# A sort's digit table shared between two engines, and a new order of the steps around it, in a kernel of retention and two mixtures of experts

## The chip, the cores and the metric

The kernel runs on one core of a Trainium2 chip. The metric is the device time of one execution in microseconds; lower is better. Five engines work side by side, each through its own list of instructions in order: TensorE (PE, products), VectorE (DVE), ScalarE (ACT), GpSimd (POOL), and SyncE (SP), which here only issues transfers. They wait for each other by semaphores.

## What is computed

Three stages, each on the output of the one before:

```python
# 1. retention: per head, over 768 steps, batch 4, 8 heads of 64
state = gamma * state + outer(k[t], v[t]);  y[t] = scale * q[t] @ state
# 2. soft mixture of experts, x: 3072 x 512, 8 experts with 4 slots each
d = softmax(x @ phi, over tokens);  c = softmax(x @ phi, over slots)
slot_out[e] = relu((d.T @ x)[e] @ w1[e]) @ w2[e];  x = c @ slot_out
# 3. noisy top-2 of 8 experts on the new x
noisy = x @ w_gate + log1p(exp(x @ w_noise)) * noise
for the two best experts of each token, with weights from a softmax of the two:
    out[token] += weight * relu(x @ w1b[e]) @ w2b[e]
```

## The kernel before

The tokens of stage 2 lie in 24 tiles of 128. Because x of stage 3 is `c @ slot_out`, with 32 slots, the first product of each expert of stage 3 is folded into a 32 x 1024 matrix, called SW: `sw_product(e)` (P0 to P7) multiplies slot_out with w1b[e] on TensorE as soon as SP's load of that matrix lands. ACT finds each one's size in `sw_sums(e)` (Abs with a sum), POOL takes the maximum over partitions for experts 0 to 3 and for 4 to 7 (`sw_all_sum`), and DVE makes power-of-two scales of it (`sw_scales(0)`, `sw_scales(1)`). ACT then writes the high half in f16 (`sw_high`), DVE the low half (`sw_low`), and TensorE spreads both to all partitions (`sw_spread_parts(e)`) in 16 units, two for each expert. The units go through three PSUM banks in turn, so unit n waits until unit n-3 has been copied to SBUF (`sw_keep`, by ACT for units 0 to 7 and the even ones after, by DVE for 9, 11, 13 and 15; `sw_kept` says on which semaphore to wait).

Beside this the routing is worked out. Each of the 6144 (token, choice) pairs gets a position in 55 tiles of 128 rows, ordered by expert. Positions are turned into a gather list, idx, by a counting sort on TensorE: DVE splits each position into a high digit (0 to 54) and a low digit (0 to 127), makes one-hot tables of both (`eq_all` and `eq_hi` of the high, `eq_lo` of the low in three parts of 16 columns of pairs, 128x2048 each), and `sort_rows(0)` to `sort_rows(2)` multiply them, 16 products each, into bank 7. Three small DVE operations make idx of it. The records of all pairs (c in f16, weight, output row) have been written to DRAM by POOL before. When idx and the second all-reduce of SW are there, POOL issues `fetch_records(0)` to `(10)`, one indirect DMA for each tile.

DVE also works out in which order the experts' w2b are used (`order_expert`, with `order_ready`). SP waits for it at the end of its list of loads, to load w2b of the third expert, 2 MB (`load_w2b(EARLY)`, L463); later ones wait for tiles too.

Then the 55 tiles: ACT stages the record's c (`stage_c`, L1102), TensorE turns it (`turn_c`, L898), ACT copies it (`keep_ct`, L1108), `hidden_b` (L921) multiplies with SW, ACT and DVE take the positive part as high and low f16 (`h_high` L1113, `h_low` L1546), `out_b` (L938) multiplies with w2b, 24 products of 512 columns a tile, DVE scales (`keep_y` L1560) and POOL writes (L576) and adds (L582) rows to the output.

Each engine's order is written out by hand. Around the change it is, on TensorE: P6, sort_rows(0), P7, units 0 to 3, sort_rows(1) and (2), units 4 to 7, units 8 and 9, turn_c(0), units 10 to 15, hidden_b(0). On ACT: sw_sums(2) to (5), the scaled eq_hi (L1088), sw_high(0) to (3), sw_sums(6) and (7), copies of units 0 to 7, sw_high(4) to (7), stage_c(0), unit 8, keep_ct(0), stage_c(1), units 10, 12, 14, h_high(0). On DVE: digits (L1479), eq_all, eq_hi, sw_scales(0), eq_lo[0], sw_low(0) to (3), eq_lo[1] and [2] (L1491), idx (L1499 to L1503), sw_scales(1), the order (L1508 to L1514), sw_low(4), and so on. On POOL: records to DRAM, two all-reduces (L560), the fetches (L570).

Of the kernel before, what the change touches and what calls it, by code (L numbers as in the profile page):

```python
# [5 lines left out]
P = 128  # L6
F32 = mybir.dt.float32
F16 = mybir.dt.float16
I32 = mybir.dt.int32
ALU = mybir.AluOpType  # L10
# [5 lines left out]
def build_program(nc, chunks, phi, w1a, w2a, w_gate, w_noise, noise, w1b, w2b, consts, out, dims):  # L16
# [3 lines left out]
    NT = B * NC  # L20
# [36 lines left out]
    with ExitStack() as ctx:  # L57
        def sb(name, shape, dt):
            return ctx.enter_context(nc.sbuf_tensor(name, shape, dt))

        def sem(name):
            return ctx.enter_context(nc.semaphore(name))
# [147 lines left out]
        digit = sb("digit", [P, 2, 2 * NT], F16)  # L210
        count_i = r_region[:, 4 * SZ + 2 * E * NT:4 * SZ + 2 * E * NT + P].bitcast(I32)
# [115 lines left out]
        eq_lo_ready = sem("eq_lo_ready")  # L327
        idx_done = sem("idx_done")
# [55 lines left out]
        def sw_kept(unit):  # L384

            if unit < 8 or unit % 2 == 0:
                return sw_act_kept, unit + 1 if unit < 8 else unit // 2 + 5
            return sw_dve_kept, (unit - 7) // 2
# [117 lines left out]
        def _(pool):  # L506
# [55 lines left out]

            for group in SW_GROUPS:
                sw_all_sum(*group)
# [22 lines left out]
            top = pool.to_reg(TOP)  # L587
# [23 lines left out]
        def _(pe):  # L611
# [251 lines left out]
            def sort_rows(part):  # L863
                if part == 0:
                    pe.wait_ge(eq_hi_ready, 1)
                    pe.wait_ge(eq_row_ready, 1)
                pe.wait_ge(eq_lo_ready, part + 1)
                for j in range(part * LO_PART, (part + 1) * LO_PART):
                    last = nc.tensor.matmul(bank[7][:, 0:2 * RT], eq_lo[part][:, j % LO_PART, :], eq_hi[:, j, :, :].rearrange("p v i -> p (v i)"),
                                            start=(j == 0), stop=(j == 2 * NT - 1), skip_group_check=True)  # L870
                if part == 2 * NT // LO_PART - 1:
                    last.then_inc(idx_done, 1)
# [14 lines left out]
            sw_product(7)  # L887
# [4 lines left out]
            sort_rows(2)  # L892
            sw_spread_parts(2)
# [87 lines left out]
        def _(act):  # L981
# [102 lines left out]
            for e in range(2, 6):  # L1084
                sw_sums(e)

# [5 lines left out]
            sw_sums(6)  # L1092
            sw_sums(7)
            for unit in range(8):
                sw_keep(unit)
            act.wait_ge(sw_scale_ready, 2)
            for e in range(4, E):
                sw_high(e)

# [20 lines left out]
            stage_c(1, 1, rec_arrival(1))  # L1120
            for unit in range(10, 2 * E, 2):
                sw_keep(unit)
            h_high(0, 0)
# [26 lines left out]
        def _(dve):  # L1150
# [328 lines left out]
            link(nc.vector.tensor_copy(digit[:, :, :], digit_i[:, :, :, :].rearrange("p d k t -> p d (k t)")))  # L1479
            by_hi = [P, 2 * NT, RT]  # L1480
# [9 lines left out]
            for j in range(0, 2 * NT, LO_PART):  # L1490
# [3 lines left out]
                if j == 0:  # L1494
                    for e in range(4):
                        sw_low(e)

            dve.wait_ge(idx_done, 1)
# [8 lines left out]
            numbers = count[0:1, 0:E]  # L1507
            link(nc.vector.tensor_reduce(order_e[:, 0, :], ahead[0:1, :, :], AX_X, ALU.add))  # L1508
            pairs = ahead_tiles[0:1, :, :]
            link(nc.vector.tensor_tensor(pairs, order_e[:, 0, :].unsqueeze(1).to_broadcast([1, E, E]),  # L1510
                                         numbers.unsqueeze(2).to_broadcast([1, E, E]), ALU.is_equal))
            link(nc.vector.tensor_tensor(pairs, pairs, numbers.unsqueeze(1).to_broadcast([1, E, E]), ALU.mult))
            link(nc.vector.tensor_reduce(order_e[:, 1, :], pairs, AX_X, ALU.add))
            nc.vector.tensor_copy(order_expert[:, :], order_e[:, 1, :]).then_inc(order_ready, 1)  # L1514
            dve.wait_ge(order_ready, 1)
# [142 lines left out]
```

## Time and profile before

| | us |
|---|---|
| median of 3 runs | 578.58 |
| lowest and highest | 577.02, 579.87 |
| the profiled execution | 580.67 |
| its span, first to last instruction | 578.9 |
| TensorE busy | 516.4 (89%) |
| VectorE busy | 284.0 (49%) |
| ScalarE busy | 188.8 (33%) |
| GpSimd busy | 254.6 (44%) |

Times in the rows are microseconds from the span's start. A row of the timeline gives start, duration, engine, line and operation, what is written and read, how many instructions were merged (x16), and in brackets how long the engine had been idle and what released it. DMA-issuing instructions of SP have the engine name SPq. In the chain of waits each row is a start, a duration and what the end of the kernel waited for in that time.

### The profile page before, as it was taken

To read this page: it belongs to the slowest core of one execution; us is meant where nothing else is said; L and a number is where in the kernel's file an instruction comes from. 1 tells how busy PE (TensorE), PEld (TensorE's weight loads), DVE (VectorE), ACT (ScalarE), POOL (GpSimd) and SP (SyncE) were. 2 spreads that over 40 slices of the span, in tenths; PEclk is the share of its full clock that TensorE was granted. 3 is DMA by queue.
4 is the path that set the end of the run, shared out by engine and by line. 5 is a ranking of instruction groups with operands and counts; after the bars stand their busy time and mean duration, and the time that the engine had idled before them with its cause. 6 is when DMAs were issued, how large, how long until landed. Compare 5 with 4: busy or idle time off the path is not lost.

```text
span 578.9 us, 13504 instructions
## 1 busy us (share of the span) xinstructions
PE 516.4 (89%) x4845; PEld 305.9 (53%) x4846; DVE 284.0 (49%) x450; ACT 188.8 (33%) x353; POOL 254.6 (44%) x216
## 2 busy tenths in 40 slices
PE   4999999997876746469999999999999999999993
PEld 4787787774474524324545454554545454545441
DVE  1666666565570488357345464546452423233330
ACT  0222222221830123546363645455322221212120
POOL 1222211211000010525558687868676666656542
PEclk9999999999985797759999999999999999999997
DMA  8899899877999996442445522222132333333410
GB/s 277 312 367 371 304 378 327 331 290 288 407 426 427 426 428 279 155 148 60 181 171 199 188 51 45 42 40 55 26 56 47 50 46 51 45 50 43 53 18 1
DMA packets 29621, 107.90 MB, mean 186 GB/s; under 512 B 11251, under 2 KB 12515, under 8 KB 24464
## 3 DMA queue, kind: packets, MB, share of 16 engines
q1 hardware_dynamic: 15408, 92.89, 41.7%
q0 software_dynamic: 14176, 14.49, 14.3%
q8 instruction: 26, 0.43, 0.3%
q14 instruction: 11, 0.09, 0.1%
HBM read 93.87 MB, written 29.43 MB: 213 GB/s over the span
## 4 chain that ended last, share of the span: by engine, by line
PE 77%; DMA 12%; DVE 4%; issue 2%; ACT 1%; another core or an unknown queue 1%; POOL 1%; SPq 0%; DVEq 0%; POOLq 0%
PE ps L938 49%; DMA w_region<-moe_w 9%; PE ps L670 4%; PE ps L921 4%; PE ps L623 4%; PE ps L664 4%; PE ps L655 3%; PE ps L677 2%; DMA s_region<-moe_w 1%; PE ps L644 1%; PE ps L808 1%; PE ps L637 1%; DMA rec_region<-records,idx 1%; PE ps L844 1%
## 5 line engine op out<-in xcount | busy, mean ns | idle before, releaser
L938 PE MATMUL ps<-w_region,s_region 128*128 (+1 forms) x1320 | 297.1, 382 | 3.7 <-ACT s_region L1113 3.6
L938 PEld LDWEIGHTS ps<-w_region,s_region 128*128 128x128 f16 x1320 | 127.2, 98 | 149.5 <-issue 10.0
L1546 DVE SCALAR_TENSOR_TENSOR s_region<-ps,s_region 128x1024 f16<-128x1024 f32 x55 | 67.4, 1225 | 156.3 <-ACT s_region L1113 150.9
L1113 ACT ACTIVATE s_region<-ps 128x1024 f16<-128x1024 f32 x55 | 56.3, 1023 | 194.7 <-PE ps L921 136.8
L576 POOL DMA_INDIRECT out<-s_region,rec_region x41 | 54.5, 1330 | 53.5 <-DVE s_region L1560 51.5
L582 POOL DMA_INDIRECT out<-s_region,rec_region x42 | 67.8, 1615 | 15.2 <-issue 12.3
L570 POOL DMA_INDIRECT rec_region<-records,idx x55 | 57.6, 1047 | 20.4 <-issue 20.4
L511 POOL TENSOR_TENSOR s_region<-w_region,s_region 128x512 f32<-128x512 f32 x22 | 22.9, 1042 | 89.2 <-PE ps L677 73.7
L921 PEld LDWEIGHTS ps<-s_region,sw_region 128*128 (+1 forms) x440 | 29.5, 98 | 14.9 <-issue 2.1
L1560 DVE TENSOR_SCALAR s_region<-ps,rec_region,y_scale 128x512 f32<-128x512 f32 x42 | 33.8, 804 | 5.7 <-PE ps L938 4.1
L921 PE MATMUL ps<-s_region,sw_region 128*128 128x128 f16 x440 | 34.0, 221 | 1.7 <-issue 1.7
L1161 DVE TENSOR_TENSOR sw_region<-ps,s_region 128x512 f32<-128x512 f32 x24 | 16.6, 691 | 34.2 <-PE ps L670 34.2
L1332 DVE SCALAR_TENSOR_TENSOR w_region<-w_region,w2b_scale 128x2048 f16<-128x2048 f32 x12 | 28.0, 2345 | 2.1 <-ACT w_region L1024 2.1
L808 PE MATMUL ps<-w_region,sw_region 128*32 128x128 f32 x448 | 19.2, 348 | 8.1 <-DMA w_region<-moe_w 7.6
L844 PE MATMUL ps<-w_region,slot_out_t 128*32 128x256 f32 x224 | 17.5, 465 | 10.1 <-DMA w_region<-moe_w 9.5
L576 POOL DMA_INDIRECT out<-r_region,rec_region x13 | 18.2, 1401 | 17.6 <-DVE r_region L1560 16.8
L1024 ACT ACTIVATE w_region<-w_region,w2b_scale 128x2048 f16<-128x2048 f32 x12 | 23.8, 2001 | 4.3 <-DVE w2b_scale L1326 4.3
L556 POOL DMA_DIRECT2D records<-rec_region x1 | 0.7, 742 | 53.4 <-DVE rec_region L1457 53.4
L984 ACT ACTIVATE s_region<-ps 128x128 f32<-128x128 f32 x24 | 6.7, 277 | 51.9 <-PE ps L637 51.9
L1039 ACT ACTIVATE r_region<-w_region 128x2048 f16<-128x2048 f32 (+1 forms) x14 | 23.3, 1666 | 0.1
L582 POOL DMA_INDIRECT out<-r_region,rec_region x13 | 20.7, 1592 | 4.5 <-issue 4.5
L808 PEld LDWEIGHTS ps<-w_region,sw_region 128*32 128x32 f32 x448 | 16.8, 141 | 10.5 <-DMA w_region<-moe_w 9.2
(239 smaller groups left out, 589.6 us busy)
## 6 DMA issues: line engine op xcount, KB each, us to landing
w_region<-moe_w SPq DMA_DIRECT2D x19, 2048.0 KB, 23.4
w_region<-chunks SPq DMA_DIRECT2D x34, 512.0 KB, 6.6
w_region<-moe_w SPq DMA_DIRECT2D x14, 1024.0 KB, 8.8
sw_region<-chunks SPq DMA_DIRECT2D x12, 512.0 KB, 6.2
s_region<-moe_w SPq DMA_DIRECT2D x3, 2048.0 KB, 22.0
s_region<-moe_w SPq DMA_DIRECT2D x2, 1024.0 KB, 8.2
s_region<-moe_w SPq DMA_DIRECT2D x1, 1536.0 KB, 6.4
out<-s_region,rec_region POOLq DMA_INDIRECT x83
```

What stands on the lines that cost most here:

```text
L570: nc.gpsimd.indirect_dma_start(rec_i[:, i * RW:(i + 1) * RW], None, records[:, :], bass.IndirectOffsetOnAxis(ap=idx[:, i:i + 1], axis=0), ...
L576: nc.gpsimd.indirect_dma_start(out[:, :], bass.IndirectOffsetOnAxis(ap=rec_i[:, i * RW + SL + 1:i * RW + SL + 2], axis=0), y_sb[i % DEPTH] ...
L582: nc.gpsimd.indirect_dma_start(out[:, :], bass.IndirectOffsetOnAxis(ap=rec_i[:, i * RW + SL + 2:i * RW + SL + 3], axis=0), y_sb[i % DEPTH] ...
L808: last = nc.tensor.matmul(bank[5][j * SL:(j + 1) * SL, 0:P], h1_blocks[:, at:at + SL], w[:, f, j * P:(j + 1) * P], start=(e == 0 and f == ...
L921: last = nc.tensor.matmul(bank[2 + 2 * r + f // 4][:, f % 4 * P:(f % 4 + 1) * P], sw_parts[:, bass.ds(e, 1), f * P:(f + 1) * P].rearrange( ...
L938: last = nc.tensor.matmul(bank[6 + r], h[:, r, f, :], w2b_parts[:, bass.ds(o, 1), part, f, :].rearrange("p e m -> p (e m)"), start=(first ...
L1024: nc.scalar.activation(w2b_parts[:, e, 0, chunks, :], w2b_in[e].rearrange("p (c m) -> p c m", c=FC)[:, chunks, :], ACT.Copy, scale=w2b_sca ...
L1039: nc.scalar.activation(unused, w2b_in[e][:, part * UNIT // parts:(part + 1) * UNIT // parts], ACT.Abs, accum_out=w2b_sum[:, 0, e, part:par ...
L1113: nc.scalar.activation(h_hi[:, r, :, :].rearrange("p c t -> p (c t)").rearrange("p (a n) -> p a n", a=2), ps[:, 2 + 2 * r:4 + 2 * r, :], A ...
L1332: last = nc.vector.scalar_tensor_tensor(out=w2b_parts[:, e, 1, chunks, :], in0=w2b_in[e].rearrange("p (c m) -> p c m", c=FC)[:, chunks, :] ...
L1546: nc.vector.scalar_tensor_tensor(out=h_lo[:, r, :, :].rearrange("p c t -> p (c t)").rearrange("p (a n) -> p a n", a=2), in0=ps[:, 2 + 2 * ...
L1560: nc.vector.tensor_scalar(y_sb[r], bank[6 + u % 2], rec[:, bass.ds(i * RW + SL, 1)], y_scale[:, bass.ds(o, 1)], ALU.mult, ALU.mult).then_i ...
```

## The change

- DVE makes parts 0 and 1 of the low digit's table. Part 2 is made on ACT: for each of its 16 columns |count - digit| in f16 (Abs with the negated digit as bias), then Relu(1 - that) over all 2048, which is 1 where the two are equal. DVE writes the negated digits (`digit_minus`); three new semaphores join the two. On ACT this stands between sw_sums(4) and sw_sums(5).
- TensorE: sw_product(7) moves from ahead of units 0 to 3 to behind sort_rows(2).
- ACT: the copies of units 0 to 3 stand ahead of sw_sums(7), unit 4 behind it, unit 6 behind sw_high(7). Units 5 and 7 are copied by DVE, behind sw_scales(1).
- DVE: the five operations of the experts' order stand ahead of the wait for the sort.
- ACT: stage_c(1) stands behind the copies of units 10, 12 and 14.
- POOL: the register load of TOP stands ahead of the wait for idx.

```diff
-            if unit < 8 or unit % 2 == 0:
-                return sw_act_kept, unit + 1 if unit < 8 else unit // 2 + 5
-            return sw_dve_kept, (unit - 7) // 2
+            if unit < 4 or unit % 2 == 0:
+                return sw_act_kept, unit + 1 if unit < 4 else unit // 2 + 3
+            return sw_dve_kept, (unit - 3) // 2
...
+            top = pool.to_reg(TOP)
             for group in SW_GROUPS:
                 sw_all_sum(*group)
...
-            top = pool.to_reg(TOP)
             for i in range(2 * DEPTH + 3):
                 fetch_records(i)
...
-                pe.wait_ge(eq_lo_ready, part + 1)
+                if part < 2:
+                    pe.wait_ge(eq_lo_ready, part + 1)
+                else:
+                    pe.wait_ge(eq_last_ready, 1)
...
             sort_rows(0)
-            sw_product(7)
             pe.wait_ge(sw_lo_ready, 4)
             sw_spread_parts(0)
             sw_spread_parts(1)
             sort_rows(1)
             sort_rows(2)
+            sw_product(7)
             sw_spread_parts(2)
             sw_spread_parts(3)
...
-            for e in range(2, 6):
+            for e in range(2, 5):
                 sw_sums(e)
+
+            act.wait_ge(digits_ready, 1)
+            for j in range(LO_PART):
+                last = nc.scalar.activation(eq_lo[2][:, j, :], count[:, :], ACT.Abs, bias=digit_minus[:, j:j + 1])
+            last.then_inc(gaps_ready, 1)
+            act.wait_ge(gaps_ready, 1)
+            nc.scalar.activation(eq_lo[2], eq_lo[2], ACT.Relu, scale=-1.0, bias=1.0).then_inc(eq_last_ready, 1)
+            sw_sums(5)
...
             sw_sums(6)
+            for unit in range(4):
+                sw_keep(unit)
             sw_sums(7)
-            for unit in range(8):
-                sw_keep(unit)
+            sw_keep(4)
             act.wait_ge(sw_scale_ready, 2)
             for e in range(4, E):
                 sw_high(e)
+            sw_keep(6)
...
             keep_ct(0, 0)
-            stage_c(1, 1, rec_arrival(1))
             for unit in range(10, 2 * E, 2):
                 sw_keep(unit)
+            stage_c(1, 1, rec_arrival(1))
...
+            nc.vector.tensor_scalar(digit_minus[:, :], digit[:, 0, 2 * LO_PART:3 * LO_PART], -1.0, None,
+                                    ALU.mult).then_inc(digits_ready, 1)
...
-            for j in range(0, 2 * NT, LO_PART):
+            for j in range(0, 2 * LO_PART, LO_PART):
...
-            dve.wait_ge(idx_done, 1)
...
-            sw_scales(1)
             numbers = count[0:1, 0:E]
...
             dve.wait_ge(order_ready, 1)
+            dve.wait_ge(idx_done, 1)
...
+            sw_scales(1)
+            sw_keep(5)
+            sw_keep(7)
             sw_low(4)
```

## Rows read from the trace of the kernel before

**Rows 1.** The page, the chain that ended last, by engine and by line
```profile
PE 77%; DMA 12%; DVE 4%; issue 2%; ACT 1%; another core or an unknown queue 1%; POOL 1%; SPq 0%; DVEq 0%; POOLq 0%
PE ps L938 49%; DMA w_region<-moe_w 9%; PE ps L670 4%; PE ps L921 4%; PE ps L623 4%; PE ps L664 4%; PE ps L655 3%; PE ps L677 2%; DMA s_region<-moe_w 1%; PE ps L644 1%; PE ps L808 1%; PE ps L637 1%; DMA rec_region<-records,idx 1%; PE ps L844 1%
```
**Rows 2.** The chain of waits in order of time: start, us, what
```profile
237.55 6.83 DMA rec_region<-records,idx
...
246.95 5.06 another core or an unknown queue
252.04 1.03 ACT s_region L1113
253.21 6.26 PE ps L938 x16
259.97 5.18 PE ps L938 x24
```
**Rows 3.** The timeline of TensorE, 223 to 249
```profile
223.30 2.57 PE L844 MATMUL ps<-w_region,slot_out_t 128*32 128x256 f32 x32 [2.26 <-DMA w_region<-moe_w]
225.80 1.65 PE L869 MATMUL ps<-r_region,s_region 128*128 128x110 f16 x16
229.19 1.93 PE L844 MATMUL ps<-w_region,slot_out_t 128*32 128x256 f32 x32 [1.74 <-DMA w_region<-moe_w]
231.05 0.85 PE L857 MATMUL ps<-s_region,r_region 128*64 128x256 f16 x12
...
232.53 1.78 PE L869 MATMUL ps<-r_region,sw_region 128*128 128x110 f16 x32
...
239.95 1.49 PE L857 MATMUL ps<-s_region,r_region 128*64 128x256 f16 x12
245.25 1.49 PE L857 MATMUL ps<-s_region,r_region 128*64 128x256 f16 x12 [3.81 <-ACT sw_region L1061]
248.45 1.01 PE L921 MATMUL ps<-s_region,sw_region 128*128 128x128 f16 x8 [1.71 <-issue]
```
**Rows 4.** The timeline of VectorE, 215 to 248
```profile
215.03 0.21 DVE L1479 CAST digit<-r_region 128x96 f16<-128x96 int32 x1
...
226.33 4.48 DVE L1491 TENSOR_TENSOR sw_region<-count,digit 128x2048 f16<-128x2048 f16 x2
...
234.85 0.21 DVE L1503 SCALAR_TENSOR_TENSOR idx<-ps,r_region 128x55 int32<-128x55 f32 x1
...
236.62 0.16 DVE L1514 CAST order_expert<-order_e 1x8 int32<-1x8 f32 x1
...
241.66 0.47 DVE L1466 SCALAR_TENSOR_TENSOR s_region<-ps,sw_scale,s_region 128x256 f16<-128x256 f32 x1
...
247.66 0.69 DVE L1473 CAST sw_region<-ps 128x512 f16<-128x512 f32 x1 [1.04 <-issue]
```
**Rows 5.** The timeline of ScalarE, 221 to 240
```profile
221.09 0.38 ACT L1051 ACTIVATE s_region<-ps 128x256 f32<-128x256 f32 x1 [6.11 <-PE ps L844]
...
221.46 2.54 ACT L1088 ACTIVATE r_region<-s_region,row 128x2640 f16<-128x2640 f16 x1
223.90 1.55 ACT L1055 ACTIVATE s_region<-ps,sw_scale 128x256 f16<-128x256 f32 x4
...
239.30 0.31 ACT L1102 ACTIVATE s_region<-rec_region 128x128 f16<-128x128 f16 x1 [1.09 <-DMA rec_region<-records,idx]
```
**Rows 6.** The timeline of GpSimd and of SyncE's queue, 231 to 238
```profile
231.74 0.38 POOL L560 PARTITION_ALL_REDUCE sw_sum<-sw_sum  x1 [13.41 <-ACT s_region L1051]
236.10 1.14 POOL L570 DMA_INDIRECT rec_region<-records,idx  x1 [3.98 <-issue]
...
237.81 0.35 SPq L463 DMA_DIRECT2D w_region<-moe_w  x1
```
**Rows 7.** Stretches: us; busy PE, PEld, DVE, ACT, POOL; PEclk; DMA share; GB/s
```profile
228.00:236.00 8.00, 6.02 (x96) 4.18 (x96) 4.25 (x11) 3.73 (x9) 0.38 (x1) 1.00 0.01 2
...
242.00:244.00 2.00, 0.00 (x0) 0.00 (x0) 0.14 (x1) 0.00 (x0) 1.45 (x2) 0.50 1.01 428
```
**Rows 8.** Groups of ScalarE's instructions by line: busy, mean ns, idle before
```profile
L1078 ACT ACT_TABLE_LOAD x1 | 1.3, 1283 | 0.0
```

More of the change, by code:

```diff
@@ L210, in build_program @@
         digit = sb("digit", [P, 2, 2 * NT], F16)
+        digit_minus = sb("digit_minus", [P, LO_PART], F32)
         count_i = r_region[:, 4 * SZ + 2 * E * NT:4 * SZ + 2 * E * NT + P].bitcast(I32)
@@ L327, in build_program @@
         eq_lo_ready = sem("eq_lo_ready")
+        digits_ready = sem("digits_ready")
+        gaps_ready = sem("gaps_ready")
+        eq_last_ready = sem("eq_last_ready")
         idx_done = sem("idx_done")
@@ L1496, in _ @@
                         sw_low(e)
-            dve.wait_ge(idx_done, 1)
-            link(nc.vector.tensor_scalar(idx_part[:, 0, :], bank[7][:, 0:RT], 0.0, float(RECORDS + 2 * NT), ALU.is_equal,
-                                         ALU.mult))
-            link(nc.vector.scalar_tensor_tensor(out=idx_part[:, 1, :], in0=bank[7][:, 0:RT], scalar=float(2 * NT),
-                                                in1=idx_part[:, 0, :], op0=ALU.mult, op1=ALU.add))
-            nc.vector.scalar_tensor_tensor(out=idx[:, :], in0=bank[7][:, RT:2 * RT], scalar=-float(2 * NT),
-                                           in1=idx_part[:, 1, :], op0=ALU.add, op1=ALU.add).then_inc(idx_ready, 1)
-            sw_scales(1)
             numbers = count[0:1, 0:E]
@@ L1515, in _ @@
             dve.wait_ge(order_ready, 1)
+            dve.wait_ge(idx_done, 1)
+            link(nc.vector.tensor_scalar(idx_part[:, 0, :], bank[7][:, 0:RT], 0.0, float(RECORDS + 2 * NT), ALU.is_equal,
+                                         ALU.mult))
+            link(nc.vector.scalar_tensor_tensor(out=idx_part[:, 1, :], in0=bank[7][:, 0:RT], scalar=float(2 * NT),
+                                                in1=idx_part[:, 0, :], op0=ALU.mult, op1=ALU.add))
+            nc.vector.scalar_tensor_tensor(out=idx[:, :], in0=bank[7][:, RT:2 * RT], scalar=-float(2 * NT),
+                                           in1=idx_part[:, 1, :], op0=ALU.add, op1=ALU.add).then_inc(idx_ready, 1)
+            sw_scales(1)
+            sw_keep(5)
+            sw_keep(7)
             sw_low(4)
```

## Prediction

> **What bounds the kernel now.** I read the page first: of the chain that ended last, 77% is TensorE and 49% L938 alone, the product of the output tiles [rows 1]. Its 55 tiles run back to back from the first one on (24 products in 5.18 us from 259.97, and so on to the end [rows 2]), so whatever moves the start of tile 0's L938 moves the end by as much, and nothing else in this change touches what follows. Next I read the chain of waits in order of time, ahead of that start: record 1's fetch (6.83 us), then 5.06 us that end in no release that the profile can name, then ACT's L1113 (h_high of tile 0), then L938 at 253.21 [rows 2]. Then the four engines and SP from 214 to 253, instruction by instruction. The reader is to see a queue that is held at its head: ACT issues in order, and its stage_c(1) stands ahead of the copies of units 10, 12 and 14. Record 1 lands at 237.55 + 6.83 = 244.38, though unit 10 was through TensorE when the group of 239.95 had done its first four products. TensorE restarts the last three units only at 245.25 and reaches hidden_b(0) (L921) at 248.45 [rows 3]. Ahead of that, the sort ends at 232.53 + 1.78 = 234.31 [rows 3], DVE makes idx by 235.06 [rows 4], POOL starts fetch 0 at 236.10 and record 0 is used at 239.30 [rows 5, 6].
>
> **The last third of the digit table on ACT.** DVE loses one of the two L1491 of the pair at 226.33, 2.24 us [rows 4], and gains one 128x16 negation of about 0.1 to 0.2 us right after the digit copy of 215.03 [rows 4]. ACT gains 16 Abs of 128 columns, a wait on itself, and one Relu of 2048 columns. It has idled 6.11 us up to 221.09 [rows 5], for w1b[5]'s product. Start: digits at 215.03 + 0.21, the negation, so 215.5. No row has this Abs with its bias. The nearest are stage_c, 0.31 us for 128 columns alone, and the four L1055 with a scale operand, 1.55 us for four of 256 columns, 0.39 each. Back-to-back ones overlap, so the bounds are 0.19 (half of the wider one) and 0.39; I take 0.28, a little under the row of the same width: 16 x 0.28 = 4.5, to 220.0. Relu: 2.54 x 2048/2640 = 1.97 by L1088 [rows 5], to 222.0. So sw_sums(5) starts 0.9 us late; by the bounds the table ends at 220.5 (no delay) to 223.7 (2.6 late). The Trainium skill, ScalarE: Activation LUTs, What ACT_TABLE_LOAD costs, says that a pointer operand for the bias adds about 93 ns and that neighbours overlap by as much; by its figures an estimate for one Abs is 0.29 us, and the sum would not change.
>
> Who waits behind it: L1088, the four sw_high of 223.90, DVE's sw_low, and DVE's second table, whose end moves from 228.57 to 229.5. Part 3's table (222.0) is no longer late for anyone.
>
> **Sort ahead of P7.** Here P6 and P7 are sw_product(6) and (7). TensorE finished sort_rows(0) at 227.45 and stood idle until w1b[7] landed, 1.74 us before 229.19 [rows 3]. In the new order it does units 0 to 3 there. Units 0 to 2 take 0.85 and unit 3 another 0.41 after a copy by ACT, as at 231.05 [rows 3], now at 227.45 to about 229.2, part of it at the lower clock. The second table ends at 229.5, so sorts 1 and 2 run 229.5 to 231.3 (1.78, at full clock: 1.00 from 228 to 236 [rows 7]). DVE's three index operations end 235.06 - 234.31 = 0.75 after the sort: idx at 232.0, against 235.06, 3.1 us earlier. The cost: P7 moves from 229.19 to 231.3 and ends at 233.2 (1.93). POOL's second all-reduce stands ahead of the fetches in its queue and needs sw_sums(7). In before it began 0.62 us after P7's end and took 0.38 [rows 3, 6]. Now that gives 234.2. So 2.2 of the 3.1 us are lost to POOL's queue. From there POOL needs 236.10 - 235.06 = 1.04 to its first fetch [rows 4, 6]; moving the register load of TOP ahead can take at most a part of that, and I count nothing: fetch 0 starts at 235.2, 0.9 earlier.
>
> **Order of experts in DVE's wait.** From idx's end at 235.06 to 236.78 DVE does nine small operations, the four of sw_scales(1) and the five of this order, so the five take some 1.0 us, now beside TensorE's sort: order_ready at 229.5 + 1.0 = 230.5 instead of 236.78 [rows 4]. Nothing on DVE waits for them. But SP has been waiting for this semaphore, and 1.03 us later, at 237.81, issued the 2 MB load of the third expert's w2b [rows 6]. It will now go at 231.5. In before the DMA engines were still full of it at 242 to 244, at 428 GB/s [rows 7], and record 1, asked for at 237.55, fell under it: 6.83 us from issue to landing, where record 0 took 239.30 - 236.10 = 3.2 including the start of stage_c. By that the load's data will now lie at about 232 to 238, so **record 0 falls under its tail**. Two readings of its landing: free of the load, 235.2 + 3.2 = 238.4; as record 1, which came 244.38 - 237.81 = 6.57 after the load's issue, 231.5 + 6.6 = 238.1. The upper bound is the whole 6.8: 242.0. I take 238.8, a little over the two that agree, so stage_c(0) gains 0.5 us (bounds: +1.4 with a table that costs no delay, to -2.7).
>
> **Copies shared anew, and stage_c(1) behind SW's copies.** Units 5 and 7 go to DVE at 0.69 each and ACT takes unit 6 behind the second sw_high. ACT's last sw_high ends about 236.7 by this plan (scales ready by 235.0, 1.59 for the four as in the group of rows 5), so units 8 and 9 are through before record 0 arrives. From stage_c(0) on, the order is that of before: units 10 to 12 start 0.65 after it (239.95 against 239.30). Then keep(10) follows at once, where before it waited for record 1. In the old clock: unit 10 done about 240.6, its copy to 241.2, unit 13 to 241.9; sw_low(7), 241.66 + 0.47 = 242.13 [rows 4], then lets unit 14 run to 242.6 and, with unit 12's copy, unit 15 to 243.05. In before they ended at 245.25 + 1.49 = 246.74 [rows 3]. That takes 3.7 us off. Record 1, fetched 1.45 us after record 0, is not needed until ACT has copied unit 14, some 4 us later, and even a 6.8 us fetch would reach h_high by less than a microsecond.
>
> **The unnamed waits.** Unit 15's products end at 246.74 but DVE's copy of it starts at 247.66, with "issue" as the only reason [rows 4]: 0.92 us. hidden_b(0) ends at 248.45 + 1.01 = 249.46, but L1113 starts at 252.04 [rows 2, 3]: 2.58 us. The change gives no reason why they should go, and the traces none why they should stay. The profiled execution took 580.67 against a median of 578.58, 2.1 more, so the timed runs may not have them in either kernel. Both ways they cancel. Bounds: 0 and 3.5 us of further gain.
>
> **The sum.** 0.5 (record 0) + 3.7 (record 1's hold gone) = 4.2 us, tile 0's L938 at 249.0 instead of 253.2. The first L938 group took 6.26 us for 16 products 0.39 each (the clock stood at 0.50, the 1.2 GHz level, at 242 to 244 [rows 7]), where the rest take 0.22. TensorE works in the same pattern ahead of it, so I count this as equal, within 1 us either way. The profiled 580.67 becomes 576.5 with a span of 574.7; applied to the median, 578.58 - 4.2 = **574.4 us**.
>
> **Rivals.**
> 1. Record 0 is held by the early w2b load as record 1 was, 6.8 us: at 242.0, stage_c(0) loses 2.7 where I count a gain of 0.5, and it stands ahead of everything else on ACT. 574.4 + 3.2 = 577.6: no change that can be told. For it: record 1 shows the effect at full size. Against it: the load will be 3.7 us old at the fetch, not 0.3 us younger.
> 2. The unnamed waits go with the new timing, in runs that had them: 3.5 us more, 570.9. For it: nothing else ended so late there. Against: no cause is known.
> 3. A small transfer is served in turn with the large one: record 0 is free of the load, at 238.4 or, with no delay by ACT's table, 237.9: 573.5 to 574. The Trainium skill, DMA: Bandwidth & Descriptors, Queues, rings and completion order, states that each DMA engine goes round its queues packet by packet, which would make an overlap cheap. The 6.83 us against 3.2 in the trace speak against it, so this gets little.
> 4. Slower: ACT's table overruns. Place: between 215.5 and P5's sums. If Abs, Relu and the return to Abs each cost a table load of 1.28 us [rows 8], and one Abs 0.39, the table ends at 215.5 + 3.8 + 6.2 + 2.0 = 227.5, 6.4 us late instead of 0.9. Sort, order, P7 and fetches shift by the 5.5 us more, and 4.2 becomes -1.3: 579.9. It decides from a delay of 5.1 us on, slower from there. By over 0.5% it would need a delay of 8 us. Against it: Abs, Copy and Relu ran before with no load between them.
>
> **Chances.** Forecast 0.45 (572.9 to 576), rival 1 0.22, rival 2 0.18, rival 3 0.10, rival 4 0.05. A measurement here tells a change from about 0.5%, 2.9 us: below 575.7 is faster. Of the forecast's cases some 0.85 lie there, of rival 1's 0.2, all of rivals 2 and 3: 0.38 + 0.04 + 0.18 + 0.10 = 0.70 faster. Slower by over 0.5% only with an overrun beyond rival 4's or a fault of a kind that I don't see: 0.04; the same: 0.26. The range leaves out half of rival 4 and the outer parts of rivals 1 and 2: 570.5 to 577.8.
>
> **What would show it.** ACT's Abs group ends by about 220 and Relu by 222, or else step one is off. Sort's end at 231.3 and idx at 232.0; P7 at 231.3; first L570 at 235.2, released by the all-reduce. L463 at 231.5, with the DMA rate high from 232 on. Landing of record 0 (start of L1102) decides between the forecast, rivals 1 and 3. No ACT idle of microseconds between stage_c(0) and unit 14. L1113 at 247.9, or 244.4 if rival 2 holds. The prediction is wrong if record 0 waits out the load's whole length, or if a new wait stands ahead of fetch 0.

## Result: 3.1 us faster, and the profile after

| | before | changed |
|---|---|---|
| median of 8 runs, us | 578.36 | 575.26 |
| lowest and highest | 576.83, 580.91 | 572.91, 576.31 |
| the profiled execution | 580.67 | 572.91 |
| its span | 578.9 | 571.2 |

The ratio of the times is 0.9935, 95% interval 0.9909 to 0.9960. The medians are 3.1 us apart (2.3 to 5.3 by the interval), where 4.2 had been forecast. The profiled executions are 7.8 us apart, more than twice as much. That of before is near the slow end of its kernel's runs and that of the changed kernel is the fastest of its own, so the profiles are read here by distances inside one execution. In the changed kernel's profile the work ahead of the change (the digit copy of DVE, 215.83 against 215.03) came 0.8 us later; distances from that copy leave this out. They hold for these two executions only: in the kernel before the path to the fetch doesn't start at that copy, but at the landing of w1b[7], for which P7 waits [rows 3]. The sections on run 9 and on the sum come back to this.

The timeline of ScalarE in the changed kernel (start, us, engine, line; L1096 is the Abs, L1099 the Relu, L1058 sw_sums, L1103 the scaled eq_hi, L1062 sw_high, L1068 the copies, L1119 stage_c, L1125 keep_ct, L1130 h_high):

```profile
216.28 4.78 ACT L1096 ACTIVATE sw_region<-count,digit_minus 128x128 f16<-128x128 f16 x16 [0.77 <-DVE digit_minus L1497]
221.10 1.91 ACT L1099 ACTIVATE sw_region<-sw_region 128x2048 f16<-128x2048 f16 x1
222.91 0.36 ACT L1058 ACTIVATE s_region<-ps 128x256 f32<-128x256 f32 x1
...
240.73 0.31 ACT L1119 ACTIVATE s_region<-rec_region 128x128 f16<-128x128 f16 x1 [2.69 <-DMA rec_region<-records,idx]
240.94 0.58 ACT L1068 ACTIVATE sw_region<-ps 128x512 f16<-128x512 f32 x1
241.48 0.28 ACT L1125 ACTIVATE s_region<-ps 128x128 f16<-128x128 f16 x1
242.06 0.60 ACT L1068 ACTIVATE sw_region<-ps 128x512 f16<-128x512 f32 x1 [0.30 <-PE ps L861]
...
246.11 1.02 ACT L1130 ACTIVATE s_region<-ps 128x1024 f16<-128x1024 f32 x1 [1.01 <-PE ps L928]
```

Against [rows 5]: the 6.11 us of idle time ahead of sw_sums(5) are filled with the table. Record 0 is used (stage_c(0)) at 240.73, against 239.30, and now ACT waits 2.69 us for it. Then nothing holds the queue: the copy of unit 10 comes 0.3 us after keep_ct, and h_high(0) starts 5.38 us after stage_c(0), where before it took 12.74.

TensorE of the changed kernel, in its new order (L848 P6 and P7, L876 the sort, L861 units, L928 hidden_b, L945 out_b):

```profile
224.12 3.51 PE L848 MATMUL ps<-w_region,slot_out_t 128*32 128x256 f32 x32 [2.44 <-DMA w_region<-moe_w]
227.56 0.98 PE L876 MATMUL ps<-r_region,s_region 128*128 128x110 f16 x16
228.47 0.84 PE L861 MATMUL ps<-s_region,r_region 128*64 128x256 f16 x12
...
230.47 1.78 PE L876 MATMUL ps<-r_region,sw_region 128*128 128x110 f16 x32 [0.49 <-DVE sw_region L1510]
232.19 1.93 PE L848 MATMUL ps<-w_region,slot_out_t 128*32 128x256 f32 x32
...
245.46 0.61 PE L928 MATMUL ps<-s_region,sw_region 128*128 128x128 f16 x8 [0.84 <-ACT sw_region L1068]
...
247.28 5.30 PE L945 MATMUL ps<-w_region,s_region 128*128 128x512 f16 x16 [1.15 <-ACT s_region L1130]
```

Against [rows 3], the idle 1.74 us ahead of P7 are used, the sort waits 0.49 us for DVE's second table, and P7 comes last. DVE's end of idx, POOL and SP's queue:

```profile
232.87 0.21 DVE L1531 SCALAR_TENSOR_TENSOR idx<-ps,r_region 128x55 int32<-128x55 f32 x1
```
```profile
234.75 0.38 POOL L564 PARTITION_ALL_REDUCE sw_sum<-sw_sum  x1 [15.54 <-ACT s_region L1058]
235.64 1.15 POOL L575 DMA_INDIRECT rec_region<-records,idx  x1 [0.51 <-issue]
```
```profile
232.49 15.79 SPq L467 DMA_DIRECT2D w_region<-moe_w  x2
```

Idx is ready at 233.08, but POOL first does the all-reduce that needs P7, so the fetch starts 2.6 us after idx (1.04 before, [rows 4, 6]). The load (L467, two issues merged in this row) now goes 3.15 us ahead of the first fetch. The chain of waits names what follows:

```profile
235.64 5.06 DMA rec_region<-records,idx
240.70 0.02 issue
240.73 0.32 ACT s_region L1119
```

Record 0 takes 5.06 us from fetch to landing and 5.09 to its use, where it took 3.2 to its use before. The stretches (busy PE, PEld, DVE, ACT, POOL; PEclk; DMA share; GB/s) show what the DMA engines did meanwhile:

```profile
234.00:236.00 2.00, 1.30 (x20) 0.72 (x16) 0.73 (x5) 0.97 (x4) 0.74 (x2) 1.00 0.67 262
236.00:238.00 2.00, 0.43 (x4) 0.18 (x4) 1.91 (x4) 2.00 (x5) 1.69 (x2) 0.90 0.96 410
238.00:240.00 2.00, 0.73 (x6) 0.19 (x4) 1.08 (x2) 0.04 (x1) 1.39 (x3) 0.50 0.68 282
```
The last of these stretches, cut in two, and the next:

```profile
238.00:239.00 1.00, 0.73 (x6) 0.19 (x4) 0.23 (x1) 0.04 (x1) 0.70 (x2) 0.50 1.15 492
239.00:240.00 1.00, 0.00 (x0) 0.00 (x0) 0.86 (x2) 0.00 (x0) 0.69 (x2) 0.50 0.21 72
240.00:242.00 2.00, 0.82 (x7) 0.64 (x9) 0.00 (x0) 1.03 (x3) 1.70 (x2) 0.50 0.20 20
```

The load's traffic is over at 239.0, 6.5 us after its issue. Record 0 lands at 240.70, 1.7 us behind that.

### The profile page after: what moved, and what is told of

It is laid out like the page before. It is cut to its first block, busy times and chain, and to the rows that moved or that the text cites. A ratio compares the mean times of both kernels' runs of the same rounds, so it can differ in the third digit from the quotient of the medians.

```text
span 571.2 us, 13520 instructions
## 1 busy us (share of the span) xinstructions
PE 514.7 (90%) x4845; PEld 302.8 (53%) x4846; DVE 282.9 (50%) x452; ACT 194.7 (34%) x368; POOL 255.0 (45%) x216
## 4 chain that ended last, share of the span: by engine, by line
PE 75%; issue 14%; DMA 3%; DVE 2%; ACT 2%; POOL 2%; SPq 0%; DVEq 0%; POOLq 0%
PE ps L945 49%; PE ps L674 4%; PE ps L928 4%; PE ps L627 4%; PE ps L668 4%; PE ps L659 3%; PE ps L681 2%; ACT r_region L1046 1%; DMA s_region<-moe_w 1%; PE ps L648 1%; PE ps L641 1%; DMA rec_region<-records,idx 1%; PE ps L703 1%; DMA w_region<-chunks 1%; DVE s_region L1190 1%
## 5 line engine op out<-in xcount | busy, mean ns | idle before, releaser
L945 PE MATMUL ps<-w_region,s_region 128*128 (+1 forms) x1320 | 295.6, 381 | 1.1 <-ACT s_region L1130 1.1
L945 PEld LDWEIGHTS ps<-w_region,s_region 128*128 128x128 f16 x1320 | 127.2, 98 | 145.3 <-issue 3.6
L1130 ACT ACTIVATE s_region<-ps 128x1024 f16<-128x1024 f32 x55 | 56.3, 1023 | 188.9 <-PE ps L928 184.6
L928 PEld LDWEIGHTS ps<-s_region,sw_region 128*128 (+1 forms) x440 | 29.1, 98 | 13.9 <-ACT sw_region L1068 1.2
L928 PE MATMUL ps<-s_region,sw_region 128*128 128x128 f16 x440 | 33.5, 219 | 0.8 <-ACT sw_region L1068 0.8
L1178 DVE TENSOR_TENSOR sw_region<-ps,s_region 128x512 f32<-128x512 f32 x24 | 16.6, 691 | 34.2 <-PE ps L674 34.2
L848 PE MATMUL ps<-w_region,slot_out_t 128*32 128x256 f32 x224 | 19.7, 513 | 6.9 <-DMA w_region<-moe_w 6.4
L812 PE MATMUL ps<-w_region,sw_region 128*32 128x128 f32 x448 | 15.8, 302 | 9.7 <-DMA w_region<-moe_w 9.1
L1171 DVE TENSOR_TENSOR sw_region<-ps,s_region 128x512 f32<-128x512 f32 x24 | 15.4, 680 | 9.6 <-PE ps L627 9.6
```

The lines of the kernel that those rows point to most:

```text
L928: last = nc.tensor.matmul(bank[2 + 2 * r + f // 4][:, f % 4 * P:(f % 4 + 1) * P], sw_parts[:, bass.ds(e, 1), f * P:(f + 1) * P].rearrange( ...
L945: last = nc.tensor.matmul(bank[6 + r], h[:, r, f, :], w2b_parts[:, bass.ds(o, 1), part, f, :].rearrange("p e m -> p (e m)"), start=(first ...
L1130: nc.scalar.activation(h_hi[:, r, :, :].rearrange("p c t -> p (c t)").rearrange("p (a n) -> p a n", a=2), ps[:, 2 + 2 * r:4 + 2 * r, :], A ...
```

## The experiments

The theory after the result: the gain is the removal of record 1's hold on ACT's queue, which SP's w2b load had caused. That hold could be removed in two ways, and the change does both: it moves stage_c(1), and it issues the load early enough for records 0 and 1 to land together. The earlier sort and fetch are given back, because the same early load now delays record 0. The rivals: the earlier sort and fetch are the gain; or the two profiles differ mostly by the unnamed waits.

Times are medians. A ratio and its interval are taken from all the runs of both kernels, so a ratio is not quite the quotient of two medians.

| run | us | its before | ratio, 95% interval |
|---|---|---|---|
| 1, before, stage_c(1) moved | 574.86 | 578.28 | 0.9938 (0.9910 to 0.9966) |
| 2, changed, stage_c(1) back | 574.29 | 578.28 | 0.9937 (0.9911 to 0.9964) |
| 3, changed, load behind record 0 | 573.14 | 578.28 | 0.9926 (0.9894 to 0.9957) |
| 4, before, order moved | 577.64 | 578.28 | 0.9979 (0.9950 to 1.0008) |
| 5, changed, table on DVE | 575.17 | 578.87 | 0.9928 (0.9897 to 0.9960) |
| 6, before, load behind record 1 | 575.15 | 578.87 | 0.9949 (0.9922 to 0.9975) |
| 7, run 3 and sw_low(7) first | 572.51 | 578.87 | 0.9897 (0.9857 to 0.9938) |
| 8, changed, P7 back | 575.79 | 578.87 | 0.9953 (0.9928 to 0.9979) |
| 10, run 1 and load behind record 0 | 578.47 | 581.21 | 0.9954 (0.9918 to 0.9991) |
| 11, changed again | 579.19 | 581.21 | 0.9983 (0.9951 to 1.0015) |
| 12, run 7 again | 576.58 | 581.21 | 0.9950 (0.9913 to 0.9987) |

The last three, and the look at before of run 9, were made on a second chip, where every kernel took 3 to 4 us more; their times are compared with each other only.

**Run 1: stage_c(1) alone, in the kernel before.**

```diff
-            stage_c(1, 1, rec_arrival(1))
             for unit in range(10, 2 * E, 2):
                 sw_keep(unit)
+            stage_c(1, 1, rec_arrival(1))
```

> Kernel before, with only stage_c(1) moved behind the copies of units 10, 12 and 14. Theory (the head of ACT's queue was held by record 1, which the w2b load kept back): everything up to stage_c(0) stays, record 0 used at 239.3, record 1 still lands about 244.4, but unit 10 is copied at once and the copies of 10 to 14 end by 243.3; h_high(0) starts 3.7 us earlier than in the kernel before with its unnamed waits alike, so 574.7 us. Rival (the gain of the whole change comes from the earlier sort and fetch): nothing here, 578.4. Rival (the unnamed waits of 0.9 and 2.6 us ahead of h_high made most of the difference of the two profiles): the medians differ by less than 1 us while the profile may show more.

Measured 574.86, 3.4 us below before. One moved line does what the whole change does. ScalarE of this run (L1102 stage_c, L1061 copies, L1113 h_high):

```profile
240.95 0.31 ACT L1102 ACTIVATE s_region<-rec_region 128x128 f16<-128x128 f16 x1 [0.97 <-DMA rec_region<-records,idx]
...
242.28 0.60 ACT L1061 ACTIVATE sw_region<-ps 128x512 f16<-128x512 f32 x1 [0.30 <-PE ps L857]
...
246.42 0.31 ACT L1102 ACTIVATE s_region<-rec_region 128x128 f16<-128x128 f16 x1 [1.53 <-DMA rec_region<-records,idx]
246.63 1.00 ACT L1113 ACTIVATE s_region<-ps 128x1024 f16<-128x1024 f32 x1
```

Record 1 is as late as before, 5.5 us behind record 0, but the copies no longer stand behind it. It now holds h_high by 0.7 us: hidden_b(0) had ended at 245.92, and h_high follows record 1 at once.

**Run 2: stage_c(1) put back, in the changed kernel** (run 1's edit reversed).

> Changed kernel, with only stage_c(1) put back ahead of the copies. In the changed kernel records 0 and 1 landed within 0.2 us of each other (240.70 and 240.88), since the w2b load had been issued before both. Theory: stage_c(1) then waits for nothing wherever it stands, and putting it back costs 0.3 us at most: 575.3 to 575.6. Rival (the new place of stage_c(1) carries the gain in the changed kernel too): 3.7 us lost, 579.

Measured 574.29, not above the changed kernel. In its profile both records are there together, so the place of stage_c(1) no longer matters:

```profile
239.54 0.31 ACT L1119 ACTIVATE s_region<-rec_region 128x128 f16<-128x128 f16 x1 [2.73 <-DMA rec_region<-records,idx]
...
240.47 0.30 ACT L1119 ACTIVATE s_region<-rec_region 128x128 f16<-128x128 f16 x1
```

Runs 1 and 2 together: in the kernel before, the place of stage_c(1) is worth the whole gain; in the changed kernel it is worth nothing that can be told.

**Run 3: the load behind record 0, in the changed kernel.**

```diff
                 if o == EARLY:
                     sp.wait_ge(order_ready, 1)
+                    sp.wait_ge(rec_first_full[0], 16)
```

> Changed kernel, with SP's w2b load of the third expert made to wait for record 0's landing as well. Theory (record 0 lands late, 5.1 us after its fetch, because the w2b load issued earlier holds it): record 0 lands 3.2 us after its fetch, about 238.9 instead of 240.7, and the end comes 1.8 us earlier, 573.4. Its price: the load then lands some 6.5 us later, about 247, when ACT wants it at 247.4, so nothing. Rival (record 0's 5.1 us are the fetch's own, with no part of the load): no gain, 575.3; or a loss of up to 1 us if the load is now late.

Measured 573.14, 5.1 us below before. POOL, then ScalarE, of this run:

```profile
234.72 1.14 POOL L576 DMA_INDIRECT rec_region<-records,idx  x1 [0.51 <-issue]
```
```profile
237.78 0.31 ACT L1120 ACTIVATE s_region<-rec_region 128x128 f16<-128x128 f16 x1 [0.66 <-DMA rec_region<-records,idx]
```

Fetch to use is 3.06 us where it was 5.09: the load was the cause of record 0's delay. The time is 2.1 us below the changed kernel's, which the ten runs can't tell for sure; run 7 comes back to it. Not foreseen: the load lands after ACT wants it, and ACT idles 1.81 us ahead of its first sum in this profile; that moves h_high of tile 1, not the copies.

**Run 4: the order of experts alone, in the kernel before.** The five operations from `numbers = ...` to the wait for order_ready stand ahead of `dve.wait_ge(idx_done, 1)`.

> Kernel before, with only the five operations of the experts' order moved ahead of DVE's wait for the sort. Theory: the w2b load is issued about 232.9 instead of 237.8; it now holds record 0 (lands 240.5 to 241 instead of 239.3, 1.4 us lost) but no longer record 1, which lands with it instead of at 244.4. Net 1.5 to 2.5 us faster, 576 to 577, though stage_c(1) still stands ahead of the copies. Rival (the load has no part in record 1's landing): record 1 at 244.4 as before and no change, 578.4. Rival (an earlier load costs record 0 its lead and gives nothing back): 1.4 us slower, 579.8.

Measured 577.64; the interval reaches from 2.9 us faster to 0.5 slower, so the time alone does not choose between the forecast, whose 576 to 577 is just missed, and the first rival. The profile does decide whether the load holds the records: record 0 came 4.83 us after its fetch instead of 3.2, and record 1 was already there 0.93 us later, where before it took 5.1. SP's queue, POOL, ScalarE:

```profile
236.22 0.35 SPq L463 DMA_DIRECT2D w_region<-moe_w  x1
```
```profile
240.57 1.14 POOL L570 DMA_INDIRECT rec_region<-records,idx  x1 [4.05 <-issue]
```
```profile
245.40 0.31 ACT L1102 ACTIVATE s_region<-rec_region 128x128 f16<-128x128 f16 x1 [2.79 <-DMA rec_region<-records,idx]
...
246.33 0.30 ACT L1102 ACTIVATE s_region<-rec_region 128x128 f16<-128x128 f16 x1
```

In this execution P7 took 3.62 us instead of 1.93, because TensorE had the lower clock from 233 to 235 (0.50), so the fetch came some 1.7 us later than it would have.

The early load alone is thus far from the whole gain. Run 2 has the same early load and the same place of stage_c(1), and besides it the rest of the change: the table on ACT, the sort ahead of P7, the new sharing of the copies. It is 3.4 us below run 4. Drawn again and again at random from the recorded runs of both, the difference of the medians lies between 0.7 and 4.9 in 95% of the draws. So the work on the sort and the copies is not worth nothing: it pays for what the early load costs record 0. Which part of it pays, no run shows, for runs 5 and 8 take out one part each and leave the others, and the sharing of the copies was never taken out.

**Run 5: the third part of the table on DVE again, in the changed kernel.** The block of Abs, wait and Relu, the negation and their semaphores go; `range(0, 2 * NT, LO_PART)` returns.

> Changed kernel, with the third part of the digit table made on DVE again (no Abs, Relu or negation; ACT goes straight to sw_sums(5)). Theory: the table on ACT delayed sw_sums(5) by 1.2 us and DVE's second table by as much, so its removal gives that back, and DVE's third table ends about 231.4, 1 us after the second one ends now. The sort ends within 0.3 us of where it does now, order_ready and the w2b load 1 us later, fetch 0 as now: 575.3, within 0.5 either way. Rival (the table on ACT is what makes the sort early, worth the 2.2 us that one table costs DVE): 577.5.

Measured 575.17 against 575.26 for the changed kernel: the table on ACT is worth nothing that can be told. The price that the forecast put on it (ACT late, DVE's second table late) eats what DVE saves: the first fetch comes 19.80 us after the digit copy, and in the changed kernel 19.81. Record 0 is used 1.1 us later after that copy (25.96 against 24.90), since the load now goes only 2.35 us ahead of the fetch; the times don't show it. In the profile the sort's last part waits 0.30 us for DVE's third table:

```profile
231.81 0.98 PE L873 MATMUL ps<-r_region,sw_region 128*128 128x110 f16 x16
233.09 0.98 PE L873 MATMUL ps<-r_region,sw_region 128*128 128x110 f16 x16 [0.30 <-DVE sw_region L1499]
```

**Run 6: the load behind record 1, in the kernel before.** Run 3's line with `rec_first_full[1]`; nothing of the change is in it.

> Kernel before, with nothing changed but that SP's w2b load of the third expert also waits for record 1's landing; stage_c(1) stays ahead of the copies. Theory (that load is what kept record 1 back from 240.8 to 244.4): record 1 lands 3.2 us after its fetch, ACT's queue is held 0.5 us at most, and the end comes 3.2 to 3.7 us earlier: 574.6 to 575.1. Rival (record 1's landing has nothing to do with the load, it comes from fetches that follow one another): 578.3, or later where the load is now late.

Measured 575.15, 3.7 us below before. Another way to the same gain, and the cleanest proof that the load held record 1, which now comes 2.50 us after its fetch. Stage_c of both records, and ACT's first sum over the expert's w2b (L1040), for which it waits:

```profile
241.11 0.31 ACT L1103 ACTIVATE s_region<-rec_region 128x128 f16<-128x128 f16 x1 [0.96 <-DMA rec_region<-records,idx]
...
241.99 0.30 ACT L1103 ACTIVATE s_region<-rec_region 128x128 f16<-128x128 f16 x1
...
251.15 1.91 ACT L1040 ACTIVATE r_region<-w_region 128x2048 f16<-128x2048 f32 x1 [3.26 <-DMA w_region<-moe_w]
```

The late load has a price, which was named with the rival: h_high of tile 1 starts 8.59 us after that of tile 0, where it is 7.33 in run 9's profile of the kernel before. So some 1.3 us of what record 1's release gives are lost again.

**Run 7: run 3 with sw_low(7) ahead of DVE's copy of unit 11.**

```diff
             sw_low(6)
-            sw_keep(11)
             sw_low(7)
+            sw_keep(11)
```

> Changed kernel with the w2b load behind record 0's landing, as in the run that gave 573.1, and with DVE's sw_low(7) ahead of its copy of unit 11. Theory: units 14 and 15 were released by sw_low(7), 0.28 us after unit 13; now by the copies of 11 and 12, 0 to 0.3 us earlier: 572.9, not to be told from 573.1, and clearly below the kernel before. Rival (DVE's order there costs the 0.6 us that a copy takes): 572.5.

Measured 572.51, 6.4 us below before, at the rival's number; 0.6 us from run 3 can't be told apart. The six units 10 to 15 now ran as one group on TensorE (238.49, 2.95 us). It is 2.8 us below the changed kernel (0.4 to 4.9, drawn as above). The gate has its price here too, for ACT waits for the load:

```profile
247.07 1.91 ACT L1047 ACTIVATE r_region<-w_region 128x2048 f16<-128x2048 f32 x1 [2.77 <-DMA w_region<-moe_w]
```

H_high of tile 1 starts 8.10 us after that of tile 0, in the changed kernel 6.95.

**Run 8: P7 ahead of units 0 to 3 again, in the changed kernel.**

```diff
             sort_rows(0)
+            sw_product(7)
             pe.wait_ge(sw_lo_ready, 4)
...
             sort_rows(2)
-            sw_product(7)
```

> Changed kernel, with P7 put back between sort_rows(0) and units 0 to 3. Theory (the first fetch waits in POOL's queue behind the all-reduce that needs P7, so sort and P7 only trade places): the sort ends about 1.8 us later, idx comes about 234.9 instead of 233.1, and is now what releases fetch 0, about 236 instead of 235.6; record 0 lands at most 0.5 us later, since the load's tail ends at the same time: 575.3 to 576. Rival (the sort ahead of P7 is worth the 1.9 us of P7): 577.2.

Measured 575.79, 0.5 us above the changed kernel and not to be told from it. What releases the fetch has changed from the all-reduce to idx, as expected:

```profile
239.93 1.14 POOL L575 DMA_INDIRECT rec_region<-records,idx  x1 [1.68 <-DVE idx L1531]
```

The fetch comes 20.94 us after the digit copy instead of 19.81, 1.1 later, since P7 took 3.24 us here, at the lower clock, instead of 1.93. Record 0 makes good a part of that: its use is 0.8 us later (25.68 against 24.90).

**Run 9: the kernel before, a second profile.**

> The kernel before, unchanged, for a second look at its profile. If the 0.9 us ahead of unit 15's copy and the 2.6 us between hidden_b(0) and h_high(0) belong to the kernel, they stand here too. If they belong to that one execution (none of the eight other profiles so far has them), hidden_b(0)'s end releases h_high within 0.05 us, and the distance from the start of stage_c(0) to h_high(0) is some 9.3 us instead of 12.7.

One execution, 579.52 us. ScalarE and TensorE:

```profile
242.63 0.31 ACT L1102 ACTIVATE s_region<-rec_region 128x128 f16<-128x128 f16 x1 [1.01 <-DMA rec_region<-records,idx]
...
247.89 0.31 ACT L1102 ACTIVATE s_region<-rec_region 128x128 f16<-128x128 f16 x1 [4.28 <-DMA rec_region<-records,idx]
...
252.12 1.02 ACT L1113 ACTIVATE s_region<-ps 128x1024 f16<-128x1024 f32 x1 [1.67 <-PE ps L921]
```
```profile
251.06 1.01 PE L921 MATMUL ps<-s_region,sw_region 128*128 128x128 f16 x8 [0.83 <-ACT sw_region L1061]
```

P7 on TensorE, then the first fetch on POOL:

```profile
232.59 1.93 PE L844 MATMUL ps<-w_region,slot_out_t 128*32 128x256 f32 x32 [1.67 <-DMA w_region<-moe_w]
```
```profile
239.50 1.14 POOL L570 DMA_INDIRECT rec_region<-records,idx  x1 [3.98 <-issue]
```

The hold by record 1 is there (4.28 us of idle time, 4.08 in the first profile of before), the unnamed waits are not. From stage_c(0) to h_high(0) it is 9.49 us. Against the 5.38 of the changed kernel that is 4.1 us.

The fetch comes 6.91 us after P7's start, as in the first profile of before (229.19 to 236.10), but only 19.27 us after the digit copy (220.23), where it was 21.07. The reason is that w1b[7] landed sooner after that copy. So in the kernel before the fetch hangs on the landing of w1b[7]. In the changed kernel it doesn't: P7 waits for nothing, and the fetch came 19.80 to 19.82 us after the digit copy in all seven profiles in which P7 stands behind the sort.

**Runs 10, 11 and 12, together on the second chip.** Run 10 is run 1 with run 3's line, 11 the changed kernel, 12 the kernel of run 7.

> Kernel before, with stage_c(1) moved behind the copies and the w2b load behind record 0's landing, and none of the work on the sort. Theory: as with stage_c(1) moved alone (574.9), but record 1 no longer comes late behind the load, which there still held h_high by 0.7 us: 574.2. What the changed kernel with the same gate has over this (573.1 and 572.5 in two forms) is what the earlier sort and fetch are worth once nothing holds record 0: 1.3 us by the start of the first fetch. Rival (the earlier sort and fetch are worth nothing): the same time as with that gate, 573.

> The changed kernel, unchanged, beside the next run on one chip. Theory: 575.3 as before.

> The kernel with the load gated and sw_low(7) first, once more, beside the changed kernel on one chip. Theory: 1.9 to 2.2 us below the changed kernel. Rival (the difference so far came from different chips): less than 1 us below it.

Run 12 is 2.6 us below run 11, close to the 2.8 of the first chip, but drawn as above that reaches from 4.5 below to 0.6 above: the gate on the load is likely worth 2 to 3 us, and each chip alone hardly proves it. Run 11's median is 2.0 us below that of before, but its interval holds 1, so here alone the change is not proved. Run 10, 2.7 us below before, is not the 4 us that were forecast for it in the first chip's numbers, and 1.9 above run 12, where 1.3 to 1.7 had been expected as the worth of the earlier fetch. Twelve runs each can't tell that 1.9 either. What run 10 was to tell (whether the gate helps once stage_c(1) is moved) stays open.

The unnamed waits are back in the profiles of these three. ScalarE and TensorE of run 11:

```profile
244.91 0.30 ACT L1119 ACTIVATE s_region<-rec_region 128x128 f16<-128x128 f16 x1
250.12 1.02 ACT L1130 ACTIVATE s_region<-ps 128x1024 f16<-128x1024 f32 x1 [4.92 <-remote]
```
```profile
246.64 1.01 PE L928 MATMUL ps<-s_region,sw_region 128*128 128x128 f16 x8 [3.17 <-issue]
```

Stage_c(0) was at 239.52, so 10.6 us to h_high(0), where the other profile of the same kernel has 5.38. They come and go in one and the same program. They do not mark a slow execution: this one took 577.23 us, the second fastest of run 11's twelve.

## Why the prediction was right, and where it was off

**What bounds the kernel.** Right in the main: the tiles run back to back from tile 0 on, and what starts tile 0 sooner ends the kernel sooner. But the rest is not quite the same. From h_high(0) to the end it is 326.9 and 325.6 us in the two profiles of before, 325.1 in that of the changed kernel, and from 324.8 to 326.8 in the others. Part of it is the first group of L938, which the forecast had counted as equal within 1 us: 6.26 and 5.68 us before, 5.30 changed.

**The table on ACT.** 16 Abs were put at 4.5 us and took 4.78, the Relu at 1.97 and took 1.91. Sw_sums(5) was to be 0.9 us late and started 1.2 after P5's end. The spacing of the Abs is (4.78 - 0.39)/15 = 0.293 us, 0.39 being the mean duration of one in the profile. The estimate by the figures of the Trainium skill, ScalarE: Activation LUTs, What ACT_TABLE_LOAD costs, was 0.29, and the trace agrees. Rival 4 is out: no table load stands in the group. Run 5 adds what the forecast did not say outright: with all its costs this edit is worth nothing here.

**Sort ahead of P7.** Idx was to come 3.1 us earlier. From the digit copy it took 233.08 - 215.83 = 17.25 us instead of 20.03: 2.8. Against run 9 (18.24) it is only 1.0. That POOL's queue takes most of it back was right: the fetch starts 19.81 us after the digit copy instead of 21.07, 1.3 earlier, where 0.9 was forecast. Against run 9 (19.27) it is 0.5 later. What the forecast left out is that in before the fetch hangs on the landing of w1b[7], so that the worth of the earlier sort changes from execution to execution. Then POOL now needs 0.51 us from the end of the all-reduce to the fetch and not 1.04. Run 8 separates the two reasons one could think of: there the register load stands ahead too, but idx is what POOL waits for, and it takes 239.93 - 238.96 = 0.97. So the register load is worth 0.07 us at most, and the rest is that the waits for idx are already fulfilled. Run 8 also shows that with P7 back the time is the same within the measurement.

**The early load.** Order_ready and the issue came as forecast: 1.02 us apart, the load 3.15 us ahead of the fetch (3.7 forecast). The term that was mis-sized is **record 0's landing**. I took 3.6 us of the 3.2 to 6.8 that bounded it, and it was 5.06. So stage_c(0), forecast 0.5 us earlier than before, came 240.73 - 215.83 = 24.90 after the digit copy instead of 24.27: 0.6 later. I had shifted record 1's 6.57 us after the load's issue to record 0, as if the two transfers only had to end together. Record 1 did land as the load's traffic ended. Record 0, asked for in the middle of that traffic, landed only after it. The last column is the distance from the end of the traffic, taken as the last quarter of a microsecond above 200 GB/s, which is 6.5 to 7.0 us after the load's issue in every one of these profiles:

| run | load issued ahead of the fetch, us | fetch to use, us | landing behind the load's traffic, us |
|---|---|---|---|
| before, record 0 | -1.7 | 3.2 | |
| before, record 1 | -0.3 | 6.9 | -0.2 |
| 9, record 1 | -0.3 | 6.9 | -0.3 |
| 1, record 1 | -0.3 | 7.1 | 0.1 |
| 5, record 0 | 2.35 | 6.16 | 1.7 |
| changed, record 0 | 3.15 | 5.09 | 1.7 |
| 11, record 0 | 3.15 | 5.05 | 1.4 |
| 8, record 0 | 4.28 | 4.74 | 2.5 |
| 4, record 0 | 4.35 | 4.83 | 2.7 |
| 3, record 0, load behind it | | 3.06 | |

Rival 1, record 0 held as record 1 was, was thus half true: 1.9 of its 3.6 us. And of the two signs by which the forecast was to be called wrong, the first did come: record 0 waited until the load's traffic was over, and 1.7 us more. That the measured time lies near the forecast does not make this step right. Rival 3 is out: the overlap is not cheap. The rule behind it, from the Trainium skill, DMA: Bandwidth & Descriptors, Queues, rings and completion order, that an engine goes round its queues packet by packet, may still hold for each packet. That a small transfer is then hardly delayed does not follow from it, since 3.2 us became up to 7.1.

**The hold on ACT's queue.** Right, and shown by runs 1 and 6. Forecast 3.7 us. By run 9 against the changed kernel it is 9.49 - 5.38 = 4.1; run 1, where it is alone, gives 3.4 us of time, run 6 gives 3.7.

**The unnamed waits.** They were taken as equal in both kernels, and rival 2 priced their going at 3.5 us. Medians show no such gain, and runs 9 and 11 show why: before has executions without them, and the changed kernel has executions with them. Of the 7.8 us between the profiled pair they make 12.74 - 9.49 = 3.25; another 1.8 lies behind h_high(0). Their cause is open. They stand around hidden_b(0), each behind products of TensorE, they appeared in four of the fourteen profiles (before, 10, 11, 12), three of those on the second chip.

**The sum.** -0.6 (record 0 later) + 4.1 (hold gone) = 3.5, against 3.1 measured. But the first term is from the first profile of before and the second from run 9's. From the digit copy to h_high(0) the changed kernel took 30.28 us. Run 9 alone took 31.89, which makes 1.6, and the first profile 37.01, which makes 6.7 with the unnamed waits in it. With 5.06 for 3.6 the forecast's own sum would have been 4.2 - 1.5 + 0.4 for the earlier fetch = 3.1, but the hold and the first group of L938, some 0.4 and 0.4 to 1.0 us better than forecast, are not in that. That it meets the measured 3.1 so well is luck: the terms are known to about 1 us, and the time to 2.3 to 5.3.

A version that beats both by its medians: run 7, and on the second chip run 12. The 2 MB load waits for the record that everyone needs first. Record 0 is then used 23.03 us after the digit copy in run 7, where it was 24.90 in the changed kernel.

## What to carry to other kernels

Ahead of a wait that stands in an in-order queue, ask what stands behind it that doesn't need it; here one line moved behind three copies was worth as much as the whole rearrangement. Before an operation is moved earlier, look who is waiting for it: the order of experts cost DVE nothing, but released a 2 MB load into the path of a gather of 128 rows of 35 words. Two remedies for one wait do not add, so take each alone before paying for both. And a distance between two points of a profile says something only if the later one hangs on the earlier one: here the fetch of the kernel before hung on a load's landing, not on the digit copy.

## What the runs showed of the hardware that was not expected

- The first gather of 128 rows that POOL issues took 3.06 to 3.2 us to its use with no load's traffic around it (the second 2.50 us in run 6), and 4.7 to 7.1 us with a 2 MB load of SP issued up to 4.4 us before or 0.3 us after it. The delay is largest when the load is issued together with the gather, not when it is half done. A gather issued with the load landed within 0.4 us of the end of the load's traffic, one issued 2.35 to 4.35 us after the load 1.4 to 2.7 us behind that end.
- POOL's first gather started 0.51 us after the operation ahead of it where the waits for idx were already fulfilled, and 0.97 (run 8) to 1.04 us (before) after idx where it waited.
- The engines around hidden_b(0) stood 3 to 5 us longer with no release that the profile names, in some executions of a program and not in others (12.74 and 9.49 us from stage_c(0) to h_high(0) in the kernel before, 5.38 and 10.60 in the changed one).
